# Seven block products in place of eight for the second layer's input product, on one core

## What is computed

```python
x = attention(q, k, v).reshape(2304, 512)
h = x @ w_in                      # 2304 x 2048
x = (s * relu(h) ** 2 + b) @ w_out
h = x @ w2_in
out = (h / (1 + exp(-1.702 * h))) @ w2_out
```

## Time and profile before

| | |
|---|---|
| median of three runs | 1066.96 us |
| the profiled execution | 1063.62 us |
| its span in the profile | 1061.8 us |
| busy in the span: PE, DVE, ACT, POOL | 1020, 641, 609, 747 us |
| attention until about | 529 us |
| first layer alone, then second layer | 529 to 653, 653 to 1061.8 us |

### The profile page before, as it was taken

How to read it: one execution, slowest core, us unless ns; L and a number is a source line. 1 busy time by engine, 2 the same in 40 slices (tenths; PEclk the granted TensorE clock), 3 DMA queues, 4 the chain that set the end, 5 groups by cost and what they waited for, 6 DMA issues and landing times.

```text
span 1061.8 us, 17879 instructions
## 1 busy us (share of the span) xinstructions
PE 1020.1 (96%) x5824; PEld 904.5 (85%) x5824; DVE 641.0 (60%) x1486; ACT 608.7 (57%) x1157; POOL 747.2 (70%) x708
## 2 busy tenths in 40 slices
PE   5878999999999999999999999999999999999998
PEld 4657888888888888888889999999999999999997
DVE  7898999899999998999345554322222222222222
ACT  6766666666666665765454556545454454554543
POOL 5648997787788887876556566676676676666663
PEclk9998999999999999999999999999999999999999
DMA  6127978887977789778734444444335454454441
GB/s 189 48 79 205 228 191 210 206 231 204 240 187 188 186 223 220 193 183 202 190 110 131 127 121 120 120 132 155 121 119 167 122 164 122 119 167 121 150 137 51
DMA packets 107611, 169.42 MB, mean 160 GB/s; under 512 B 11392, under 2 KB 72960, under 8 KB 107520
## 3 DMA queue, kind: packets, MB, share of 16 engines
q1 hardware_dynamic: 107520, 168.28, 58.3%
HBM read 128.12 MB, written 4.72 MB: 125 GB/s over the span
## 4 chain that ended last, share of the span: by engine, by line
PE 69%; DVE 17%; SPq 6%; DMA 4%; issue 3%; ACT 1%; ACTq 0%; DVEq 0%
PE y_ps L620 29%; PE scores L601 24%; DVE scores L693 5%; PE shared L601 5%; DVE prob L719 5%; SPq L444 5%; PE scores L573 4%; PE scores L516 4%; DVE blocks L733 3%; DMA w_raw<-slabs 2%; DMA q_raw<-q 1%; PE shared L573 1%; DVE gate L750 1%; DVE g_lo L760 1%; DVE limit L700 1%
## 5 line engine op out<-in xcount | busy, mean ns | idle before, releaser
L1031 POOL TENSOR_TENSOR w_lo<-w_raw,win_hi 128x512 fp32r<-128x512 f32 x192 | 277.3, 1444 | 91.5 <-ACT win_hi L876 88.7
L1038 POOL TENSOR_TENSOR w_lo<-w_raw,wout_hi 128x512 fp32r<-128x512 f32 x192 | 247.4, 1288 | 103.5 <-ACT wout_hi L883 103.3
L753 DVE TENSOR_TENSOR gate<-scores,gate 128x384 f32<-128x384 f32 x96 | 53.5, 557 | 298.8 <-ACT gate L893 298.8
L620 PE MATMUL y_ps<-wout_hi,g_lo 128*128 128x512 f32 x576 | 226.9, 394 | 0.0
L620 PE MATMUL y_ps<-w_lo,g_hi 128*128 128x512 f32 x576 | 226.7, 394 | 0.0
L620 PE MATMUL y_ps<-wout_hi,g_hi 128*128 128x512 f32 x576 | 226.3, 393 | 0.0
L840 ACT ACTIVATE prob<-scores,neg_max 128x576 f32<-128x576 f32 (+1 forms) x160 | 118.5, 741 | 124.1 <-DVE scores L693 118.7
L601 PE MATMUL scores<-act_hi,w_lo 128*128 128x384 f32 x492 | 166.1, 338 | 0.0
L601 PE MATMUL scores<-act_hi,win_hi 128*128 128x384 f32 x492 | 165.7, 337 | 0.0
L601 PE MATMUL scores<-act_lo,win_hi 128*128 128x384 f32 x492 | 165.3, 336 | 0.0
L1025 POOL TENSOR_SCALAR prob<-prob,row_inv 128x576 f32<-128x576 f32 (+1 forms) x160 | 125.4, 796 | 26.4 <-DVE row_inv L707 26.3
(11 more groups left out here) (73 smaller groups left out, 1703.8 us busy)
## 6 DMA issues: line engine op xcount, KB each, us to landing
w_raw<-slabs SPq DMA_DIRECT2D x190, 512.0 KB, 3.7
prob_t<-blocks SPq DMA_DIRECT2D x96, 120.0 KB, 3.1
k_raw<-k SPq DMA_DIRECT2D x32, 288.0 KB, 5.1
q_raw<-q SPq DMA_DIRECT2D x48, 192.0 KB, 4.2
prob_t<-blocks SPq DMA_DIRECT2D x96, 96.0 KB, 3.1
v_sb<-v SPq DMA_DIRECT2D x26, 320.0 KB, 5.4
prob_t<-blocks SPq DMA_DIRECT2D x96, 80.0 KB, 4.0
prob_t<-blocks SPq DMA_DIRECT2D x96, 64.0 KB, 3.7
```

The source lines that it names most:

```text
L620: mm = nc.tensor.matmul(y_ps[g][:], gp[:, n % 2, toks], wp[:, :], start=(f == 0 and k == 0), stop=(f == SLABS - 1 and k == 2))
L1031: nc.gpsimd.tensor_tensor(in_of(w_lo, n), in_of(w_raw, n), win_hi[n % IN_HI][:].bitcast(F32), ALU.subtract).then_inc(win_lo_ready, 1)
L1038: nc.gpsimd.tensor_tensor(out_of(w_lo, n), out_of(w_raw, n), wout_hi[n % OUT_HI][:].bitcast(F32), ALU.subtract).then_inc(wout_lo_ready, 1)
```

## The change

The first layer keeps its 96 steps. Its first four tiles (`ROW_TILES`) are made and turned as before. The output product of its last two tiles is computed feature-major by `output_chunk`: four chunks of 128 features with the weights stationary and 384 tokens moving, 12 matmuls of 384 for 9 of 512, so that these tiles need no transposes. The activations of the second layer are kept raw (`x_raw`), and their high and low parts are made later, by `b_tick`.

The second layer runs in 24 groups `d` (3 pairs of tiles x 8 pairs of slabs). The 2 x 2 blocks of a group (two slabs by two tiles, each summed over the 512 model features in two halves of 256) are made by the Winograd form of Strassen's scheme: seven products of half the depth, 6 matmuls each, in place of eight. It needs sums of weight blocks (`a_sums` on DVE, four of 256 columns per group), sums of activation blocks (`b_tick`, per pair of tiles), and seven sums of products (`sum_up` on DVE), of which four are the blocks of h. For each block follow ACT's sigmoid (`gate_block`), DVE's product with h, ACT's high part (`high_block`) and DVE's low part (`low_block`). The output product of group `d - 1` stands between the products of `d`, in four pieces of 9 matmuls (`units_behind`), of which each group of 3 signals for itself. The loads are issued by SP one group ahead: `load_a`, `load_o`.

```diff
-STEPS = LAYERS * LAYER_TILES * SLABS
+STEPS = LAYER_TILES * SLABS
+ROW_TILES = 4
...
-H_RING = 4
+H_RING = 3
...
+PRODUCTS = [(True, A11, B11), (False, A12, B21), (True, T2, S2), (False, T3, S3), (True, T1, S1), (False, A22, S4),
+            (True, T4, B22)]
...
+TWIN_BLOCKS = [(0, 0), (1, 1), (1, 0), (0, 1)]
...
+            def load_a(d):
+                if d >= 2:
+                    sp.wait_ge(product_ready, PRODUCT_COUNT * (d - 1))
+                sp.dma_start(a_raw[:, d % 2, :, :], twin_in[d % TWIN_SLABS]).then_inc(a_loaded[d % 2], 16)
...
+            for d in range(1, TWINS + 1):
+                if d + 1 < TWINS:
+                    load_a(d + 1)
+                    load_o(d + 1)
+                if d >= TWIN_SLABS and d % TWIN_SLABS == 0:
+                    for tile in range(2):
+                        for g in range(GROUPS):
+                            store(d // TWIN_SLABS - 1, tile, g)
...
+            def output_chunk(n, c):
...
+                for k, (wp, gp) in enumerate(((hi, g_hi), (hi, g_lo), (lo, g_hi))):
+                    mm = nc.tensor.matmul(chunk_bank(c)[:, 0:TOK], wp[:, feats], gp[:, n % 2, :],
+                                          start=(f == 0 and k == 0), stop=(f == SLABS - 1 and k == 2))
...
+            def product(d, n):
...
+                pe.wait_ge(a_lo_ready, 3 * d + (1 if a in (A11, A12) else 2 if a == A22 else 3))
...
+                elif n == 0:
+                    pe.wait_ge(h_summed, H_SUMS * (d - 1) + H_C12 + 1)
...
+                elif n == 1:
+                    pe.wait_ge(h_summed, H_SUMS * (d - 1) + H_C21 + 1)
+                elif n == 2:
+                    pe.wait_ge(product_kept, d + 1)
+                else:
+                    pe.wait_ge(h_summed, H_SUMS * d + (H_C11, H_U2, H_U3, H_C22)[n - 3] + 1)
+                for c in range(2):
...
+                    for k, (wp, xp) in enumerate(((hi, x_hi), (hi, x_lo), (lo, x_hi))):
+                        mm = nc.tensor.matmul(twin_bank(x), wp, xp, start=(c == 0 and k == 0),
+                                              stop=(c == 1 and k == 2))
...
+            for d in range(TWINS):
+                product(d, 0)
+                units_behind(d, 0)
+                product(d, 1)
+                product(d, 2)
+                units_behind(d, 1)
+                product(d, 3)
+                product(d, 4)
+                units_behind(d, 2)
+                product(d, 5)
+                product(d, 6)
+                units_behind(d, 3)
...
+            def a_sums(d):
...
+                nc.vector.tensor_tensor(sums[:, 0, :], half[1][0], half[0][0], ALU.subtract).then_inc(a_sum_ready, 1)
+                nc.vector.tensor_tensor(sums[:, 2, :], half[1][1], half[1][0], ALU.subtract).then_inc(a_sum_ready, 1)
+                dve.wait_ge(a_sum_ready, SUMS * d + 1)
+                nc.vector.tensor_tensor(sums[:, 1, :], half[1][1], sums[:, 0, :], ALU.subtract
+                                        ).then_inc(a_sum_ready, 1)
+                dve.wait_ge(a_sum_ready, SUMS * d + 3)
+                nc.vector.tensor_tensor(sums[:, 3, :], half[0][1], sums[:, 1, :], ALU.subtract
+                                        ).then_inc(a_sum_ready, 1)
...
+            def sum_up(d, n):
...
+                nc.vector.tensor_tensor(place, twin_bank(PRODUCTS[product][0]), kept[:, term, :], ALU.add
+                                        ).then_inc(h_summed, 1)
...
+            def low_block(d, i):
+
+                dve.wait_ge(g2_hi_ready, BLOCK_COUNT * d + i + 1)
+                nc.vector.tensor_tensor(g2_lo[:, i, :], gate2[:, i % 2, :], g2_hi[:, i, :].bitcast(F32),
+                                        ALU.subtract).then_inc(g2_lo_ready, 1)
...
+                nc.scalar.copy(a_hi[:, d % 2, T1:T4 + 1, :], a_sum[:, d % 2, :, :]).then_inc(a_hi_ready, 1)
...
+                nc.gpsimd.tensor_tensor(a_sum_lo[:, d % 2, :, :], a_sum[:, d % 2, :, :],
+                                        a_hi[:, d % 2, T1:T4 + 1, :].bitcast(F32), ALU.subtract
+                                        ).then_inc(a_lo_ready, 1)
...
+                nc.gpsimd.tensor_tensor(o_lo[:, d % 2, :, :], o_raw[:, d % 2, :, :],
+                                        o_hi[:, d % 2, :, :].bitcast(F32), ALU.subtract).then_inc(o_lo_ready, 1)
```

More of the change, by code:

```diff
@@ L255, in turn_due @@
     done, f = n // SLABS - 1, n % SLABS
-    if not 0 <= done < LAYER_TILES:
+    if not 0 <= done < ROW_TILES:
         return None
@@ new lines, in unit @@
+            def unit(d, i, g):
+                f, tile = TWIN_BLOCKS[i]
+                pair, e = d // TWIN_SLABS, d % TWIN_SLABS
+                if g == 0:
+                    pe.wait_ge(g2_lo_ready, BLOCK_COUNT * d + i + 1)
+                    if i == 0:
+                        pe.wait_ge(o_lo_ready, d + 1)
+                if e == 0 and i < 2:
+                    if pair > 0:
+                        pe.wait_ge(z_copied, 2 * GROUPS * (pair - 1) + GROUPS * tile + g + 1)
+                    elif tile == 1:
+                        pe.wait_ge(x_chunks_ready, DC + g + 2)
+                    elif g == GROUPS - 1:
+                        pe.wait_ge(x_chunks_ready, DC + 1)
+                    else:
+                        pe.wait_ge(square_ready, STEPS)
+                toks = slice(g * P, (g + 1) * P)
+                hi, lo = o_hi[:, d % 2, f, :], o_lo[:, d % 2, f, :]
+                for k, (gp, wp) in enumerate(((g2_hi, hi), (g2_lo, hi), (g2_hi, lo))):
+                    mm = nc.tensor.matmul(z_bank(tile, g), gp[:, i, toks], wp,
+                                          start=(e == 0 and i < 2 and k == 0),
+                                          stop=(e == TWIN_SLABS - 1 and i >= 2 and k == 2))
+                mm.then_inc(unit_done, 1)
@@ new lines, in units_behind, with steps_output @@
+            def units_behind(d, i):
+                for g in range(GROUPS):
+                    if d > 0:
+                        unit(d - 1, i, g)
+                    else:
+                        n, c = divmod(i * GROUPS + g, DC)
+                        output_chunk(STEPS - OUT_LAG + n, c)
+            def steps_output(n):
+                if n // SLABS < ROW_TILES:
+                    output(n)
+                else:
+                    for c in range(DC):
+                        output_chunk(n, c)
@@ L664, in _ @@
                 mlp(beat - MLP_FROM)
-            for s in range(FIRST_PURE, STEPS + OUT_LAG):
+            for s in range(FIRST_PURE, STEPS):
                 if turn_due(s) is not None:
@@ L989, in _ @@
                 if s + 2 < STEPS:
                     slab_in_hi(s + 2)
+                if s == A_FROM:
+                    a_plain_hi(0)
+                    a_sums_hi(0)
+            for d in range(TWINS):
+                if d > 0:
+                    high_block(d - 1, 3)
+                if d == 1:
+                    copy_chunk(STEPS - 1, 0)
+                keep(d)
+                if d == 1:
+                    for c in range(1, DC):
+                        copy_chunk(STEPS - 1, c)
+                if pair_ends(d - 2):
+                    for g in range(GROUPS):
+                        copy_z(d - 2, 1, g)
+                for tick in ticks_in(d):
+                    b_tick(*tick)
+                gate_block(d, 0)
+                if d == 0:
+                    gated_hi(STEPS - 1)
+                high_block(d, 0)
+                out_hi(d)
+                if d + 1 < TWINS:
+                    a_plain_hi(d + 1)
+                gate_block(d, 1)
+                if d + 1 < TWINS:
+                    a_sums_hi(d + 1)
+                high_block(d, 1)
+                if pair_ends(d - 1):
+                    copy_z(d - 1, 0, 0)
+                gate_block(d, 2)
+                gate_block(d, 3)
+                if pair_ends(d - 1):
+                    copy_z(d - 1, 0, 1)
+                    copy_z(d - 1, 0, 2)
+                high_block(d, 2)
@@ L992, in _ @@
+            high_block(TWINS - 1, 3)
+            for tile in range(2):
+                for g in range(GROUPS):
+                    copy_z(TWINS - 1, tile, g)
         @block.gpsimd
@@ L1110 @@
     values = np.stack([values[key] for key, _, _ in VALUES])
+    first, second = slabs_of(moe_w_in, moe_w_out)
+    twin_first, twin_second = slabs_of(moe2_w_in, moe2_w_out)
     arrays = {
```

433 lines of the change are left out of this document (336 added, 97 removed).

## The result

| | before | changed |
|---|---|---|
| median | 1067.44 us (1062.5 to 1068.54, 4 runs) | 1112.44 us (1108.94 to 1117.81, 4 runs) |
| ratio | | 1.0427, 95% interval 1.0374 to 1.0479 |
| profiled execution, its span | 1063.62, 1061.8 us | 1110.57, 1108.8 us |
| from the start of step 95 to the end of the span | 416.1 us | 469.4 us |

Slower, as forecast, and 17 us above the predicted 1095. The interval given, 1050 to 1122, holds it, but only because it was drawn wide enough for the rival with the lower clock: the likeliest case alone ended at 1112.

The account below looks back on a forecast made before the run. TensorE bounds the second layer; terms -25.3 - 2.6 + 0.9 - 1 - 1 + 55 + 1.5 + 1 = +28.5 on 1063.62 give 1092, or 1095 us on the median's scale; range 1050 to 1122.

Parts of the forecast that it names:

- the rival with the lower clock: Second layer: both meetings, and group gaps lower the clock; +10 to +25, 1105 to 1120 us, chance 0.10.
- the likeliest case: Second layer with both meetings in each group: 1080 to 1112 us, chance 0.64.
- both meetings: Second layer, each group: VectorE's third weight sum, then block 1's low part, wait out 1024-wide GpSimd splits; chance 0.64.
- Term 6: Second layer: TensorE's product 0 starts 2.4 us late, waiting for VectorE's sums; 23 groups, +55 us, ends 0 and +76.
- Terms 1 and 2: Second layer products, 42 matmuls a group for 48: -25.3 us; transposes of two tiles dropped, 8 trios: -2.6 us.
- Term 3: Feature-major output of 32 steps, 12 matmuls of 0.176 us in place of 9 of 0.231: +0.9 us.
- Term 4: Attention: VectorE loses 18 operations of 0.42 us; -1 us, between 0 and -7.5.
- Term 5: End of the kernel: one copy of the last rows behind the last matmul in place of three; -1 us.
- Terms 7 and 8: First group, sigmoid table switch and last gated_lo in chain: +1.5 us; each of two new pairs, late a_sums: +0.5.
- One meeting only: Second layer: second alone 0.65 us a group (15 us), first alone 0.5 (11 us); 1054 to 1056 us, chance 0.12.
- No meeting: Second layer: the engines never meet and PE stays the bound; -23, 1044 us, chance 0.10.

Follow-up runs that it names:

- e2: Changed kernel with one added wait: GpSimd's 1024-wide low part of the output weights starts only behind VectorE's next four weight sums; 1038.57 us.
- e6: Changed kernel with GpSimd's two 1024-wide subtractions per group each made in four of 256 columns, orders and waits kept; 1040.61 us.
- e4: Changed kernel with one TensorE matmul repeated 8 times more just ahead of its wait for VectorE, filling the gap; 1101.28 us.
- e7: e2 with VectorE making the sum for block C21 six times in place of once; 1096.32 us.
- e11: e7 with six repeats in place of five, so seven sums for C21; 1123.22 us.
- e5: The changed kernel once more, as it is; 1115.03 us.
- e1: Changed kernel with ScalarE making the high part of the weight sums behind the block's high part instead of ahead of it; 1051.45 us.
- e9: Changed kernel with only the output weights' low part on GpSimd made in four operations of 256 columns; 1083.11 us.
- e3: Changed kernel with both the edit of e1 and the edit of e2; 1043.56 us.

## Why the prediction was right, and what it missed

- **Direction and the cause** were right, and shown: both meetings are at the operations named, groups without a half-clock stretch are 18.2 us (predicted 18.1), and with the meetings moved (e2) or cut (e6) they are 15.71 and 15.87 (predicted 15.7). What was named as the proof of the opposite, groups of 15.7 us, came as soon as one wait was added. The steps of the sum fit too: in the group that starts at 736.69 the third weight sum ends 10.9 us behind product 0, block 1's low part 17.1 and the last sum 18.1, where 10.8, 17.0 and 18.0 had been worked out.
- **Term 6** (+55) is 22 x 2.5 = 55 us in the groups, as worked out. Its upper end assumed 1.5 us of slack ahead of product 0, and it is 1.8.
- **The step that failed** is the clock: "A gap of 2.4 us per group could do this again, though it costs little while PE waits anyway", with a chance of 0.10 and left out of the sum. It does not cost little. PE stands still while it waits for VectorE, but the lower clock comes behind the wait, when PE works, and product 0, the units and product 1 then take 1.54 us longer. VectorE's next due times are set by those products, so nothing absorbs it: 14 x 1.54 = 21.6 us. e4, e7 and e11 show it by itself. The rival's own size, +10 to +25 and 1105 to 1120 us, holds the result. On the scale of the profiled executions the sum with it is 1092 + 21.6 - 3.6 (by which this profile is early at step 20) = 1110, against 1110.6. What I set against it, the clock of 1.00 behind a single gap of 1.28 us, was true and spoke only for gaps of that size; the row with 2.06 us and a clock of 0.68 was the nearer one to a gap of 2.4, and should have decided. It was also misread: in the trace of the kernel before the clock is at the lower level from 76.3 us on, before that wait ends and behind one of 1.65 us up to 74.22; and it had been there once before, behind a wait of 1.71 us.

```profile
41.25 0.53 PE L516 MATMUL scores<-k_hi,q_hl 128*128 128x288 f32 x2 [1.71 <-DVE prob L719]
...
42.20:45.60 3.40, 3.40 (x18) 2.88 (x18) 2.63 (x8) 1.76 (x4) 3.10 (x6) 0.50 0.01 2
...
74.22 0.51 PE L516 MATMUL scores<-k_hi,q_hl 128*96 128x288 f32 x2 [1.65 <-DVE prob L719]
...
76.40:77.70 1.30, 0.00 (x0) 0.00 (x0) 1.26 (x6) 0.64 (x1) 0.00 (x0) 0.50 0.01 3
```

- **Terms 1 and 2** (-25.3 and -2.6): e2's stage has plain groups of 15.71 us against four steps of 4.19 (16.76) before. Over 24 groups that is -25.2. By the 2.5 ns rule of the Trainium skill (TensorE: Matmul & The Clock Gate, § Wait — 56ns, not 53.3ns?) it would be 42 x 0.1625 + 36 x 0.216 = 14.6 us, an estimate from the page; the group measured here is 1.1 us longer. The steps that had a trio before take 4.16 instead of 4.51, so -2.8.
- **Term 3** had the wrong sign, too small to matter: a feature-major step is 4.16 us, not 4.22, so -0.9 instead of +0.9. Against it the step that starts at 588.98 takes 4.65 us, the same step before 4.19; that was not in the sum. The profile names a wait for the low part `g_lo` there, which takes 1.65 us beside a GpSimd split of 1.55 us and comes late behind ScalarE's four copies of chunks; this was not tested.
- **Term 4** (-1) is -1.3 by step 60. **Term 5** (-1) is -1.3: the span ends 3.5 us behind the start of the last matmul (1105.29) instead of 4.8 (1057.01). **Terms 7 and 8**: group 0 takes 17.71 us against 14.27 with the meetings moved, so the first group pays 3.4, 0.9 more than the plain ones (1.5 was taken); at a new pair the changed kernel shows 0.1 us (group 9: 19.88), the same kernel in e5 0.6 (group 9: 18.80), since the late load falls mostly under the first meeting as said; in e2, where that cover is gone, it costs 1.5 and 1.9 us.
- **One meeting only** was put at 0.65 us a group for the second and 0.5 for the first. (With 11 us for the first its sum is 1052, not the 1054 given as the lower end.) The first alone costs 0.44 (e1, 1051.5 us), right. For the second alone no run stands by itself: e9 has 1.82 with some 1.4 us of narrow delays ahead of it; by the table the second by itself would be 2.22 - 1.8 = 0.4, an estimate.
- **No meeting** was put at 1044 us. e2, e3 and e6, without a costly one, measured 1038.6 to 1043.6.

## What to carry to other kernels

When a change fills two engines that exclude each other, write the order of their operations out against the bounding engine's clock, and go by the longest single instruction, not by the busy shares: DVE was busy 71% of the second layer and still late by 2.5 us a group. Such a meeting is moved by one wait, put so that the long operation starts behind the last sum that the bounding engine needs, or it is cut by making the long operation narrow. And cost a repeated gap of TensorE twice: once as the gap, and once as the lower clock behind it.
